# Attention and two MLPs on one core: waits of the attention loads, and the place of one batch's block maxima

## What is computed

```python
k_sum = k.reshape(B, H, nb, block, D).max(axis=3)
v_sum = v.reshape(B, H, nb, block, D).mean(axis=3)
scores_l = scale * np.matmul(q, k.transpose(0, 1, 3, 2))
mask_l = np.abs(pos[:, None] - pos[None, :]) < window
scores_s = scale * np.einsum('bhsd,bhnd->bhsn', q, k_sum) + np.log(block)
scores_all = np.concatenate([np.where(mask_l, scores_l, -1e9), scores_s], axis=-1)
a = np.exp(scores_all - np.max(scores_all, axis=-1, keepdims=True))
a = a / (np.sum(a, axis=-1, keepdims=True) + 1e-09)
attn = np.matmul(a, np.concatenate([v, v_sum], axis=2))
...
h = np.maximum(x @ w_in, 0.0)
x = h * h @ w_out
...
h = x @ w_in2
g = (a0 + a1*h + a2*h**2 + a3*h**3) / (1 + |b0|*|h| + |b1|*h**2 + 1e-6)
out = g @ w_out2
```

## Time and profile before

| | |
|---|---|
| median of 3 runs | 594.93 us (593.92 to 596.02) |
| the profiled execution's own time | 594.87 us |
| its span in the profile | 592.8 us |
| TensorE busy | 583.8 us, 98% of the span |
| VectorE, ScalarE, GpSimd busy | 409.4, 290.5, 154.7 us |
| granted clock of TensorE | 0.9 or more of full speed in every slice |
| end of the attention stage (TensorE's last output) | about 71 us |

### The profile page before, as it was taken

One profiled execution on the slowest core, in us unless ns is written; L12 is line 12 of the kernel. 1 busy time (PEld: TensorE's weight loads), 2 busy tenths in 40 slices (PEclk: granted clock), 3 DMA queues, 4 the chain that ended last, 5 costly groups with the idle time before them and its releaser, 6 DMA issues.

```text
span 592.8 us, 10635 instructions
## 1 busy us (share of the span) xinstructions
PE 583.8 (98%) x3770; PEld 479.3 (81%) x3770; DVE 409.4 (69%) x791; ACT 290.5 (49%) x613; POOL 154.7 (26%) x159
## 2 busy tenths in 40 slices
PE   8899999999999999999999999999999999999997
PEld 6678788888888888888888888888888888888885
DVE  6788796763433233457666788888888888888885
ACT  6899511101310110311011887777777776867775
POOL 4669910000300000400000354353342212222221
PEclk9999999999999999999999999999999999999999
DMA  7786460000000000033223100000100000100001
GB/s 245 232 246 197 158 250 0 1 0 1 1 0 0 0 0 0 0 108 106 82 96 107 71 1 1 0 1 0 71 0 0 0 0 0 72 0 1 0 1 71
DMA packets 11618, 31.42 MB, mean 53 GB/s; under 512 B 1600, under 2 KB 2112, under 8 KB 11584
## 3 DMA queue, kind: packets, MB, share of 16 engines
q1 hardware_dynamic: 11296, 30.68, 15.4%
q10 hardware_dynamic: 288, 0.26, 0.1%
HBM read 27.79 MB, written 3.15 MB: 52 GB/s over the span
## 4 chain that ended last, share of the span: by engine, by line
PE 94%; DMA 3%; ACT 1%; issue 1%; DVE 0%; SPq 0%; POOL 0%
PE bank L565 44%; PE bank L633 22%; PE bank L650 22%; PE bank L551 2%; PE bank L535 2%; DMA q<-qT 2%; DMA kraw<-kT 1%; PE bank L501 1%; PE bank L521 1%; ACT prob L715 0%; PE bank L510 0%; PE bank L528 0%; POOL prob L385 0%; DVE prob L937 0%; DVE hlo L1084 0%
## 5 line engine op out<-in xcount | busy, mean ns | idle before, releaser
L565 PE MATMUL bank<-xhi,whi 128*128 (+1 forms) x384 | 149.9, 390 | 0.0
L565 PE MATMUL bank<-xhi,wlo 128*128 (+1 forms) x384 | 149.5, 389 | 0.0
L565 PE MATMUL bank<-xlo,whi 128*128 (+1 forms) x384 | 149.4, 389 | 0.0
L732 ACT ACTIVATE hsq<-bank 128x512 f32<-128x512 f32 x48 | 28.8, 600 | 213.2 <-PE bank L565 213.1
L443 POOL TENSOR_TENSOR denom<-denom,habs 128x512 f32<-128x512 f32 (+1 forms) x49 | 66.0, 1348 | 246.1 <-ACT denom L820 246.1
L565 PEld LDWEIGHTS bank<-xlo,whi 128*128 128x128 f32 x384 | 72.2, 188 | 14.8
L565 PEld LDWEIGHTS bank<-xhi,whi 128*128 128x128 f32 x384 | 72.1, 188 | 14.9
L565 PEld LDWEIGHTS bank<-xhi,wlo 128*128 128x128 f32 x384 | 72.0, 188 | 14.9
L650 PE MATMUL bank<-whi,hhi 128*128 128x512 f32 x192 | 75.0, 390 | 0.6 <-DVE hlo L1084 0.6
L1084 DVE TENSOR_TENSOR hlo<-ratio,hhi 128x512 fp32r<-128x512 f32 (+1 forms) x49 | 51.0, 1041 | 34.7 <-ACT hhi L803 34.6
L650 PE MATMUL bank<-wlo,hhi 128*128 128x512 f32 x192 | 74.7, 389 | 0.0
(11 more groups left out here) (80 smaller groups left out, 888.0 us busy)
## 6 DMA issues: line engine op xcount, KB each, us to landing
wraw<-w SPq DMA_DIRECT2D x29, 512.0 KB, 3.3
vwin<-vw SPq DMA_DIRECT2D x16, 288.0 KB, 3.7
out<-osb SPq DMA_DIRECT2D x12, 256.0 KB, 2.1
kraw<-kT SPq DMA_DIRECT2D x7, 384.0 KB, 4.6
q<-qT SPq DMA_DIRECT2D x7, 384.0 KB, 4.8
wraw<-w SPq DMA_DIRECT2D x6, 256.0 KB, 5.1
kraw<-kT SPq DMA_DIRECT2D x2, 128.0 KB, 2.9
q<-qT SPq DMA_DIRECT2D x1, 256.0 KB, 3.7
```

Of the source, the lines that this page charges most:

```text
L565: last = mm(hps[j % 2][:, :], W[a][:, j, kt * P:(kt + 1) * P], X[b][:, kt, bass.ds(CH * c, CH)], start=kt == 0 and i == 0, stop=kt == KT - ...
L732: a.activation(hsq[:, i, :], hps[i][:, :], ACT.Relu).then_inc(h_free, 1)
```

## The change

It has two parts. On SyncE, from pair-batch 3 on (`DEEP = 3`), k(n) waits for the first half of v(n-1), q(n) for the second half of v(n-1), the first half of v(n) for k(n), and the second half for q(n). For this each half of v gets its own semaphore, and `summary` waits for both. On VectorE the block maxima of pair-batch 3 leave iterations 2, 3 and 4 ahead of masked and stand behind masked(7) in iteration 3 (first part) and behind masked(8) in iteration 4 (the other two parts in one call). Those of pair-batches 4 to 7 stay where they are.

```diff
--- before.py
+++ after.py
@@ -66,6 +66,7 @@
 KP = S + 2 * BAND
 THIRD = S // GPB
 WARM = (4 * P, 2 * P)
+DEEP = 3
 SPLIT_AT = {G: divmod(G - 11, 2) for G in range(11, 11 + 4 * EARLY)}
 SUMMARY_AT = [0] + [GPB * n - 2 - (n > 1) for n in range(1, NB)]
 
@@ -171,7 +172,7 @@
     q_in = [sem(f"q_in{r}") for r in range(RING)]
     k_first = [sem(f"k_first{i}") for i in range(GPB)]
     k_in = [sem(f"k_in{r}") for r in range(RING)]
-    vw_in = [sem(f"vw_in{r}") for r in range(V_RING)]
+    vw_in = [[sem(f"vw_in{r}_{i}") for i in range(2)] for r in range(V_RING)]
     coef_in = sem("coef_in")
     w_first = [sem(f"w_first{j}") for j in range(EARLY)]
     w_second = [sem(f"w_second{j}") for j in range(EARLY)]
@@ -243,9 +244,9 @@
 
         return q_in[n % RING], 16 * (n // RING + (n % RING > 0))
 
-    def vwin_landed(n):
-
-        return vw_in[n % V_RING], 32 * (n // V_RING + 1)
+    def vwin_landed(n, i):
+
+        return vw_in[n % V_RING][i], 16 * (n // V_RING + 1)
 
     block = nc.Block()
     block.__enter__()
@@ -257,8 +258,10 @@
                 sp.wait_ge(s_done, GPB * (n - RING + 1) + 1)
             if n == 1:
                 sp.wait_ge(q_first[0], 16)
+            elif n < DEEP:
+                sp.wait_ge(*q_landed(n - 1))
             else:
-                sp.wait_ge(*q_landed(n - 1))
+                sp.wait_ge(*vwin_landed(n - 1, 0))
             sp.dma_start(kraw[n % RING][:, BAND:BAND + S], kT[n]).then_inc(k_in[n % RING], 16)
 
         def load_k_first(i):
@@ -268,6 +271,8 @@
         def load_q(n):
             if n >= RING:
                 sp.wait_ge(s_done, GPB * (n - RING + 1) + 2)
+            if n >= DEEP:
+                sp.wait_ge(*vwin_landed(n - 1, 1))
             sp.dma_start(q[n % RING][:, :], qT[n]).then_inc(q_in[n % RING], 16)
 
         def load_vwin(n):
@@ -275,12 +280,15 @@
                 sp.wait_ge(s_done, GPB * (n - RING + 2) - (n == 2))
             if n >= V_RING:
                 sp.wait_ge(o_done, done(2, GPB * (n - V_RING + 1) - 1))
-            if n > 0:
-                sp.wait_ge(*vwin_landed(n - 1))
             for i, half in enumerate((slice(0, NW // 2), slice(NW // 2, NW))):
-                if n > 0 and i == 1:
+                if 0 < n < DEEP and i == 0:
+                    for j in range(2):
+                        sp.wait_ge(*vwin_landed(n - 1, j))
+                if n >= DEEP and i == 1:
+                    sp.wait_ge(*q_landed(n))
+                elif n > 0 and (n >= DEEP or i == 1):
                     sp.wait_ge(*k_landed(n))
-                sp.dma_start(vwin[n % V_RING][0:KW, half, :], vw[n][:, half, :]).then_inc(vw_in[n % V_RING], 16)
+                sp.dma_start(vwin[n % V_RING][0:KW, half, :], vw[n][:, half, :]).then_inc(vw_in[n % V_RING][i], 16)
 
         def load_first(j):
             sp.dma_start(wraw[:, j:j + 1, 0:KT * P],
@@ -513,7 +521,8 @@
 
         def summary(n):
 
-            pe.wait_ge(vw_in[n % V_RING], 32 * (n // V_RING + 1))
+            for i in range(2):
+                pe.wait_ge(*vwin_landed(n, i))
             pe.wait_ge(sums_copied, n)
             pe.wait_ge(vsum_copied, n)
             for j in range(GPB):
@@ -1007,12 +1016,16 @@
                 (x_lo if G % 2 else x_hi)(G // 2 - 1)
             if G == 1:
                 block_max(2, 0, GPB)
-            for n in range(3, NB):
+            for n in range(4, NB):
                 part = G - GPB * (n - 2) + 1
                 if 0 <= part < GPB:
                     block_max(n, part, 1)
             if G + 4 < GROUPS:
                 masked(G + 4)
+            if G == 3:
+                block_max(3, 0, 1)
+            if G == 4:
+                block_max(3, 1, 2)
         square(0, 0)
         x_hi(XPAIRS - 1)
         x_lo(XPAIRS - 1)
```

## The result

The changed kernel takes 596.87 us (median of 12 executions, 594.83 to 600.36) against 594.70 for the kernel before on the same chip (12 executions). The ratio is 1.0051, 95% interval 1.0033 to 1.0069 (the two medians alone give 1.0036): **slower by 0.4 to 0.5%**. The forecast was 594.8 and 0.1 us faster, with a range that holds the result; a loss that is clear of the noise is not what it says.

The account below looks back on a forecast made before the run. TensorE, busy 583.8 of 592.8 us, was taken as the bound. Of the 1.73 us removed at batch 3 some 0.9 stay at output(7), and slower loads give that back by batch 7: 0.1 us faster, 594.8, range 592.8 to 598.0.

Parts of the forecast that it names:

- The wait removed: Attention stage, iteration 4: VectorE's wait for k of batch 3 goes, and with it TensorE's loss of 1.73 us.
- Two under way, not three: SyncE's loads from batch 3 on: the waits leave two transfers under way, where the change's title says three.
- The price of a late k: Attention stage: output(3n-5) cannot start before batch n's k has landed plus 3.56 us.
- The landings: k of batches 3 to 7 lands at 20.7, 27.8, 34.9, 42.2 and 49.5 us.
- the sum's term of 7.1 us a batch: Loads from batch 3 on: k 3.7, half of v 3.3 and 0.1 for issues, against TensorE's 6.85 us.
- 0.2 for each load of weights: Attention-stage loads: each 256 KB load of weights in between adds 0.2 us to k's landing times.
- 0.45 us for 0.1 us a batch: Loads: each 0.1 us more a batch costs 0.45 us at the end, over four and a half batches.
- rival 2: Loads: two transfers cost what three or four cost; 8.4 us a batch, output(16) 6 us late, 600.9 us; chance 0.23.
- Rival 1: Loads: two transfers hardly disturb each other; 6.5 us a batch, 1.7 to 2.0 us gained, 593.1 or 592.8; chance 0.27.
- the rule that stands ahead of the rivals: Trainium skill's transfer price, about 2.0 us plus bytes over 436 GB/s: 5.6 us a batch, 593.1 us in all.

## Why the prediction was wrong

- **The wait removed**: right for the profiled execution. Iteration 4 is back at 2.23 us, in the change and in one profile with the move alone. The 1.73 us are not all found again in a median (0.7 and 1.0 with the move alone). Pauses of TensorE of some 0.5 us that no releaser explains, and waits of 0.85 and 0.92 for `normalise` in iteration 13, take some of it in the two profiles; the kernel before has them too (0.75 at 29.48; for `normalise` 0.31 in one profile, 0.97 in the other), and I can't say why they fall where they do.
- **Two under way, not three**: right, for k, q and v; the weights of batches 5 to 7 come on top. With three, 2.2 us come back.
- **The price of a late k**, 3.56 us from the maximum to the output three iterations on: right to the hundredth, at batch 7 of two executions at full clock.
- **The landings**: for the profiled execution nearly right, and that is luck, since it is the fastest of twelve and the others differ. The maxima that waited stand at 27.96, 34.76, 41.74 and 49.57; the forecast landings were 27.8, 34.9, 42.2 and 49.5. Output(16) starts at 53.13, forecast 53.1; the profiled time is 594.83, forecast 594.8.
- **The step that failed** is the sum's term of 7.1 us a batch as the one time of the kernel. It held in the execution that was profiled first (7.2), and there k took 3.6 and half a v 3.3, where I assumed 3.7 and 3.3; in two other executions a batch took 8.1 and 8.2, with half a v at 4.0 in one and a k at 5.3 in the other. I took 3.3 from one transfer into a nearly idle queue (3.1) against a median of 3.7. Two terms stand in that sum: 7.1 for a batch, and 0.2 for each load of weights, for which I gave no row. In the three profiles of the change the steps without weights take 7.4 in the mean and those with weights 8.1, so 0.7 in place of 0.2; with a scatter of over 1 us from step to step, the split between the two terms is rough. And the effect of the spread is not even: below 6.85 us a batch nothing is gained, above it 4.5 times the excess is paid. By my own figure, 0.45 us for 0.1 us a batch, the median of 596.87 stands for 7.6, just past the 7.5 from which I had rival 2 decide. So it is rival 2's mechanism at about a third of its price (2.2 us of 6). Rival 1, which needs 3.3 for k and 3.1 for half a v, 6.5 a batch, is excluded: no profile of the change has medians under 3.6 and 3.3, or a batch under 7.2. With it goes the 5.6 a batch of the rule that stands ahead of the rivals.
- **What I left out**: the clock. I priced a late k in idle time alone. In two of the twelve timed executions of the waits-only kernel the mean granted clock was 0.994 and in four 0.997, in the change 0.994, 0.996 and 0.997 once each; 0.003 of 595 us at half the clock is 3.6 us, and loses at most 1.8. But the kernel before has it as well, in 12 of the 74 executions timed beside the experiments (3 of 34, 3 of 17, 6 of 23), against 13 of 48 with two under way. So the late loads may make it more frequent, and it is not theirs alone. The median of the change does not need it: nine of its twelve executions are at full clock, and their median is 596.25.

Why one execution's batches take 7.2 us and another's 8.1 stays open. I named the loads of instructions as one reason, and no run tells them from others.

## What to carry to other kernels

Spacing loads by waiting for the transfer two places ahead makes the time of a batch of four the sum of two latencies; set it against the time of the work before counting what a wait at one place gives back, and count the transfers under way from the waits, not from a name. Where loads and work come within a few per cent of each other, one execution's trace says little about the median: lateness adds up over the batches, and earliness doesn't once a buffer has to come free first. When the rate was short here, one more transfer under way brought the time back; a later deadline for each load showed no gain.

## What the runs showed of the hardware

- In the medians of the stretches named, k (384 KB) takes 3.1 us alone, 3.6 to 3.9 beside one other in the three profiles of the change (3.2 and 4.0 in the two experiments that keep its waits), and 4.6 in the kernel before. Half a v (288 KB) takes 2.9 alone, then 3.3 to 4.0, then 3.8. A batch takes 12.5 us with one under way and 7.2 to 8.2 with two.
- TensorE's clock fell to half behind idle pieces of 1.68 and 1.05 us (and stayed there for some 7 us) in one execution, and behind 0.65 and 1.04 in another. It stayed at full speed behind 0.40 and 1.04 in the first profile of the change, 0.41 and 1.04 before, and 0.30 and 1.04 in its profile at 597.99 (1.00 from 44 to 52 us). Late data is paid twice where it falls.
